# A new order of the sync engine's queue and of the slots, and a split of the softmax weights for three key tiles of six

## The reference, cut to what matters

```python
# q, k, v: (2, 8, 768, 64) float32, proj: (64, 6)
q_bucket = sum((q @ proj > 0) * 2**arange(6)); k_bucket likewise
scores = where(q_bucket[..., :, None] == k_bucket[..., None, :], q @ k.T / 8, -1e9)
attn = exp(scores - max(scores)); attn = attn / (sum(attn) + 1e-9)
x = (attn @ v), heads side by side            # (2, 768, 512)
x = (sigmoid(causal 5-tap convolution of x) * (x @ w_val)) @ w_out
u = x + real(fft(fft(x, axis=1), axis=2)); un = (u - mean) / sqrt(var + 1e-6)
out = u + relu(un @ w_ch1) @ w_ch2            # 512 -> 2048 -> 512
```

## Time and profile before

| | us |
|---|---|
| median of 3 runs | 784.6 |
| lowest, highest | 783.83, 794.24 |
| the profiled execution, its own time | 781.99 |
| its span, from the first to the last instruction | 780.1 |

### The profile page before, as it was taken

One profiled execution on the slowest core, in us unless ns is written; L12 is line 12 of the kernel. 1 busy time (PEld: TensorE's weight loads), 2 busy tenths in 40 slices (PEclk: granted clock), 3 DMA queues, 4 the chain that ended last, 5 costly groups with the idle time before them and its releaser, 6 DMA issues.

```text
span 780.1 us, 10303 instructions
## 1 busy us (share of the span) xinstructions
PE 701.6 (90%) x3696; PEld 647.9 (83%) x3696; DVE 418.7 (54%) x573; ACT 278.4 (36%) x424; POOL 381.9 (49%) x283
## 2 busy tenths in 40 slices
PE   2588889788888879878999999999999999999998
PEld 1388888787878778877989899998999999999897
DVE  3365578778888787797485467942122221212112
ACT  2146564455465454565352444211111111111110
POOL 1047778767878787788286697488100000000000
PEclk9589999999999999997999999999999999999999
DMA  9443645544544635111012112323010000001001
GB/s 246 116 123 98 155 118 139 129 113 107 144 113 112 158 106 129 50 31 42 17 50 61 41 42 75 88 85 95 11 40 0 0 28 13 0 0 41 1 0 41
DMA packets 33608, 57.67 MB, mean 74 GB/s; under 512 B 9232, under 2 KB 15632, under 8 KB 33568
## 3 DMA queue, kind: packets, MB, share of 16 engines
q1 hardware_dynamic: 33568, 57.14, 27.8%
HBM read 31.81 MB, written 3.24 MB: 45 GB/s over the span
## 4 chain that ended last, share of the span: by engine, by line
PE 71%; DVE 17%; DMA 4%; SPq 2%; issue 2%; POOL 2%; ACT 0%; DVEq 0%; POOLq 0%
PE psum L1057 63%; DVE max_col L808 4%; DVE neg_parts L818 2%; DMA a2k<-hash_bits 2%; DVE gate L862 1%; DVE qk_lo L794 1%; POOL p_lo L524 1%; DMA flag_dram<-a2q 1%; PE psum L1133 1%; DVE neg_rest L820 1%; PE psum L1138 1%; PE psum L1139 1%; PE psum L1135 1%; PE psum L1136 1%; DVE gate L859 1%
## 5 line engine op out<-in xcount | busy, mean ns | idle before, releaser
L524 POOL TENSOR_TENSOR p_lo<-probs,p_hi 128x768 fp32r<-128x768 f32 x96 | 190.2, 1996 | 66.4 <-ACT probs L647 65.1
L1028 DVE SCALAR_TENSOR_TENSOR h_lo<-psum,h_hi 128x384 fp32r<-128x384 f32 x64 | 35.7, 558 | 182.7 <-ACT h_hi L769 182.7
L808 DVE TENSOR_REDUCE max_col<-psum 128x1 f32<-128x768 f32 x96 | 91.6, 954 | 76.7 <-PE psum L1057 76.1
L644 ACT ACTIVATE p_hi<-psum 128x768 fp32r<-128x768 f32 x96 | 78.0, 813 | 104.6 <-PE psum L1057 103.0
L769 ACT ACTIVATE h_hi<-psum 128x384 fp32r<-128x384 f32 x64 | 31.5, 492 | 214.5 <-PE psum L1057 214.5
L1057 PE MATMUL psum<-a1k,a1q 128*128 128x384 f32 x192 | 74.2, 386 | 26.8 <-DMA a2k<-hash_bits 17.8
L1057 PE MATMUL psum<-unt_hi,w_hi 128*128 (+1 forms) x256 | 86.9, 339 | 0.0
L1057 PE MATMUL psum<-unt_lo,w_hi 128*128 (+1 forms) x256 | 86.3, 337 | 0.0
L1057 PE MATMUL psum<-unt_hi,w_lo 128*128 (+1 forms) x256 | 85.9, 336 | 0.0
L647 ACT ACTIVATE probs<-psum 128x768 f32<-128x768 f32 x96 | 77.3, 805 | 0.0
L1057 PE MATMUL psum<-w_lo,h_hi 128*128 128x512 f32 x192 | 75.9, 395 | 0.0
(11 more groups left out here) (124 smaller groups left out, 1561.6 us busy)
## 6 DMA issues: line engine op xcount, KB each, us to landing
stg_w<-in_w SPq DMA_DIRECT2D x32, 256.0 KB, 2.6
qk_raw<-in_qk SPq DMA_DIRECT2D x16, 384.0 KB, 5.1
a1k<-qk_hi SPq DMA_DIRECT2D x32, 192.0 KB, 5.1
flag_b<-flag_dram SPq DMA_DIRECT2D x16, 384.0 KB, 3.9
v_raw<-in_v SPq DMA_DIRECT2D x16, 192.0 KB, 3.0
a1q<-qk_hi SPq DMA_DIRECT2D x16, 192.0 KB, 4.7
a2q<-qk_hi SPq DMA_DIRECT2D x16, 192.0 KB, 5.3
a1q<-qk_lo SPq DMA_DIRECT2D x16, 192.0 KB, 5.0
```

The source lines that it names most:

```text
L524: pool.tensor_tensor(p_lo[i % PBUF][:, :], probs[i % PBUF][:, :], bits(p_hi[i % PHBUF][:, 0:S]), ALU.subtract).then_inc(p_lo_ready, 1)
L644: act.activation(halves(p_hi[i % PHBUF][:, 0:S]), ring[ring_st(i) % 2], ACT.Exp, scale=SCALE).then_inc(p_hi_ready, 1)
L808: dve.tensor_reduce(max_col[:, i % T:i % T + 1], s_ps, AX.XY, ALU.max).then_inc(max_done, 1)
L1028: dve.scalar_tensor_tensor(h_lo[:, half], psum[:, j % 2, 0:HALF], 0.0, bits(h_hi[:, half]), ALU.max, ALU.subtract).then_inc(h_lo_ready, 1)
```

## The change

What it does, by part:

1. **Split tiles.** Only tiles 1, 3 and 5 of a head (`SPLIT`) keep the six-matmul form. The others (0, 2, 4) are two plain float32 matmuls, with `probs` (now with the column of ones, PCOLS wide) as the moving operand and `v1`, float32 v with its ones, as the stationary one. Those tiles have no `p_hi` exponential and no `p_lo`. `vh` and `vl` keep three tiles of 128 columns.
2. **v.** The load of v writes straight into `v1`, in pieces of 64 columns (256 bytes), one head ahead in place of two. `v1` lies where slots 6 and 7 of `gate` will be, so the convolution of these waits for `pv_done`.
3. **Slots.** S_LEAD 10 to 11, FIRST -20 to -21; the hash at g % 12 = 9 (was 10); `max_parts` at g % 6 = 0 (was 1); `hi_qk`, `lo_qk`, `sign_bits`, `scale_kbits` one or two slots earlier; `hi_v`, `lo_v`, `reciprocals` one slot later; the convolution starts four slots later.
4. **scale_x** runs a head later, at g % 6 = 2 of head n + 2.
5. **SP.** `spread_flag` and `spread_rec` are each cut in two: the store goes out first (`store_flag` at g % 6 = 5, `store_rec` at 4), the broadcast one head's boundary later. `stack_bits` moves from g % 12 = 0 to 11, ahead of the flag. `load_qk` moves from 10 of the pair before (three pairs ahead) to 2 (two pairs ahead).
6. **After the loop.** `reciprocals(15)` comes before `gate_values(0, 0)`, and four taps of gate slot 6 (two before) come behind it, after `lo_x(1, c)`.

```diff
-ST_LEAD, S_LEAD = 2, 10
-FIRST = -20
+ST_LEAD, S_LEAD = 2, 11
+FIRST = -21
+SPLIT = (1, 3, 5)
...
             def load_v(n):
+                par = n % 2
                 if n >= 2:
-                    sp.wait_ge(vh_ready, n - 1)
                     sp.wait_ge(vl_ready, n - 1)
-                sp.dma_start(v_raw[n % 2][:, :], v[n // H, n % H, :, :].rearrange("(p t) d -> p (t d)", t=T)).then_inc(v_loaded[n % 2], 16)
+                    sp.wait_ge(pv_done, T * (n - 1))
+                sp.dma_start(tiles(v1[par][:, :])[:, :, par * D:(par + 1) * D],
+                             v[n // H, n % H, :, :].rearrange("(p t) d -> p t d", t=T)).then_inc(v_loaded[par], 16)
...
-            for g in range(FIRST, UNITS + T):
+            for g in range(FIRST, UNITS + 2 * T + 3):
                 pair, n = g // (2 * T), g // T
-                if g % (2 * T) == 10 and 0 <= pair + 3 < NPAIR and pair + 3 >= RAWS // 2:
-                    load_qk(2 * (pair + 3))
-                    load_qk(2 * (pair + 3) + 1)
+                if g % T == 1 and 1 <= n <= NH:
+                    fold_den(n - 1)
+                    if n + 1 < NH:
+                        load_v(n + 1)
+                if g % T == 4 and 1 <= n <= NH:
+                    store_rec(n - 1)
+                if g % T == 0 and 2 <= n <= NH + 1:
+                    spread_rec(n - 2)
                 if g % (2 * T) == 6 and 0 <= pair + 2 < NPAIR:
                     stack(2 * (pair + 2))
                 if g % (2 * T) == 10 and 0 <= pair + 2 < NPAIR:
                     stack(2 * (pair + 2) + 1)
-                if g % (2 * T) == 0 and 0 <= pair + 1 < NPAIR:
-                    stack_bits(pair + 1)
...
+                if g % (2 * T) == 11 and 0 <= pair + 2 < NPAIR:
+                    stack_bits(pair + 2)
+                if g % T == 5 and 0 <= n + 1 < NH:
+                    store_flag(n + 1)
+                if g % T == 1 and 0 <= n < NH:
+                    spread_flag(n)
+                if g % (2 * T) == 2 and 2 <= pair + 2 < NPAIR:
+                    load_qk(2 * (pair + 2))
+                    load_qk(2 * (pair + 2) + 1)
+                if g % T == 3 and 2 <= n + 2 < NH:
+                    load_wa(n + 2)
...
                 n = g // T
-                if 0 <= g + 1 < UNITS:
+                if 0 <= g + 1 < UNITS and is_split(g + 1):
                     lo_probs(g + 1)
-                if g % T == 3 and 0 <= n + 1 < NH:
+                if g % T == 4 and 0 <= n + 1 < NH:
                     lo_v(n + 1)
-                if g % T == 1 and 0 <= n < NH:
+                if g % T == 5 and 0 <= n < NH:
                     split_weights(n)
-                if g % T == 4 and 1 <= n <= NH:
-                    scale_x(n - 1)
+                if g % T == 2 and 2 <= n <= NH + 1:
+                    scale_x(n - 2)
...
                 act.wait_ge(st_done, i + 1)
-                act.activation(halves(p_hi[i % PHBUF][:, 0:S]), ring[ring_st(i) % 2], ACT.Exp, scale=SCALE).then_inc(p_hi_ready, 1)
+                if is_split(i):
+                    k = splits_until(i)
...
+                    act.activation(halves(p_hi[k % PHBUF][:, 0:S]), ring[ring_st(i) % 2], ACT.Exp, scale=SCALE).then_inc(p_hi_ready, 1)
...
-                if g % T == 1 and 0 <= n + 1 < NH:
+                if g % T == 0 and 0 <= n + 1 < NH:
                     max_parts(n + 1)
...
-                if g % T == 2 and 1 <= n:
+                if g % T == 3 and 1 <= n:
                     reciprocals(n - 1)
-                slot, tap = (g - 18) // (2 * T), (g - 18) % (2 * T) // 2
+                slot, tap = (g - 22) // (2 * T), (g - 22) % (2 * T) // 2
...
+                if not is_split(i):
+                    pe.wait_ge(probs_ready, i + 1)
+                    pe.matmul(first, v1[par][:, w], probs[i % PBUF][:, 0:HALF], start=start, stop=stop)
+                    pe.matmul(last, v1[par][:, w], probs[i % PBUF][:, HALF:PCOLS], start=start, stop=stop).then_inc(pv_done, 1)
+                    return
...
-                if g % (2 * T) == 10 and 0 <= pair + 2 < NPAIR:
+                if g % (2 * T) == 9 and 0 <= pair + 2 < NPAIR:
                     hash_pair(pair + 2)
```

More of the change, by code:

```diff
@@ L40, with splits_until, is_split, split_unit @@
 UNITS = T * NH
-ST_LEAD, S_LEAD = 2, 10
-FIRST = -20
+ST_LEAD, S_LEAD = 2, 11
+FIRST = -21
+SPLIT = (1, 3, 5)
+def splits_until(i):
+    return i // T * len(SPLIT) + sum(j < i % T for j in SPLIT)
+def is_split(i):
+    return i % T in SPLIT
+def split_unit(k):
+    return k // len(SPLIT) * T + SPLIT[k % len(SPLIT)]
 def turn_slot(n):
@@ L49, in hash_slot @@
 def hash_slot(pair):
-    return 2 * T * pair - 14
+    return 2 * T * pair - 15
 def turns_until(g):
@@ L186, in build @@
         assert top[0] <= wa_at
[L188 removed]
+        v1 = [at(gate_at + 4 * (NPAIR - 2) * S, "v1_0", T * P), after("v1_1", T * P)]
         assert top[0] <= gap_at
@@ L203, in build @@
         assert top[0] <= g_at
-        vh = [at(g_at, "vh0", T * P, F32R), after("vh1", T * P, F32R)]
-        vl = [after(f"vl{i}", T * P, F32R) for i in range(2)]
+        vh = [at(g_at, "vh0", len(SPLIT) * P, F32R), after("vh1", len(SPLIT) * P, F32R)]
+        vl = [after(f"vl{i}", len(SPLIT) * P, F32R) for i in range(2)]
         probs_at = top[0]
[L207 to L210, removed]
+        probs = [at(probs_at, "probs0", PCOLS)]
+        probs += [after(f"probs{i}", PCOLS) for i in range(1, PBUF)]
+        p_lo = [at(probs_at, "p_lo0", PCOLS, F32R)]
+        p_lo += [after(f"p_lo{i}", PCOLS, F32R) for i in range(1, PBUF)]
+        top[0] = max(top[0], gv_at)
         sums = [after(f"sums{i}", S) for i in range(2)]
@@ L285, in build @@
         max_rows = sem("max_rows")
-        flag_stored = sem("flag_stored")
+        flag_stored = [sem(f"flag_stored{i}") for i in range(2)]
         flag_loaded = [sem(f"flag_loaded{i}") for i in range(2)]
@@ L490, in _ @@
                 pool.memset(bits(p_hi[i][:, S + 1:PCOLS]), 0.0).then_inc(consts_ready, 1)
+            for i in range(PBUF):
+                pool.memset(probs[i][:, S:S + 1], 1.0).then_inc(consts_ready, 1)
+                pool.memset(probs[i][:, S + 1:PCOLS], 0.0).then_inc(consts_ready, 1)
             for par in range(2):
-                own, rest = (slice(D, P), slice(0, D)) if par else (slice(0, D), slice(D, P))
-                pool.memset(bits(tiles(vh[par][:, :])[:, :, rest]), 1.0).then_inc(consts_ready, 1)
-                pool.memset(bits(tiles(vl[par][:, :])[:, :, rest]), 0.0).then_inc(consts_ready, 1)
+                rest = slice(0, D) if par else slice(D, P)
+                pool.memset(tiles(v1[par][:, :])[:, :, rest], 1.0).then_inc(consts_ready, 1)
             pool.wait_ge(consts_ready, CONSTS)
@@ L997, in _ @@
                 lo_x(1, c)
+            for tap in range(1, KCONV):
+                convolve(NPAIR - 2, tap)
             for tap in range(KCONV):
@@ L1131, in weigh_v @@
                         pe.wait_ge(sums_ready, n)
-                pe.wait_ge(p_hi_ready, i + 1)
-                pe.matmul(first, vh[par][:, w], hi[:, 0:HALF], start=j == 0, stop=False)
-                pe.matmul(last, vh[par][:, w], hi[:, HALF:PCOLS], start=j == 0, stop=False)
+                if not is_split(i):
[3 more added lines that the diff above has]
+                    return
@@ L1135, in weigh_v @@
+                k = splits_until(i)
+                hi, lo = p_hi[k % PHBUF], p_lo[i % PBUF]
+                w = slice(k % len(SPLIT) * P, (k % len(SPLIT) + 1) * P)
+                pe.wait_ge(p_hi_ready, k + 1)
+                pe.matmul(first, vh[par][:, w], hi[:, 0:HALF], start=start, stop=False)
+                pe.matmul(last, vh[par][:, w], hi[:, HALF:PCOLS], start=start, stop=False)
                 pe.matmul(first, vl[par][:, w], hi[:, 0:HALF], start=False, stop=False)
-                pe.matmul(last, vl[par][:, w], hi[:, HALF:PCOLS], start=False, stop=j == T - 1)
@@ L1137, in weigh_v @@
-                pe.wait_ge(p_lo_ready, i + 1)
-                pe.matmul(first, vh[par][:, w], lo[:, 0:HALF], start=False, stop=j == T - 1)
-                pe.matmul(last[:, 0:HALF], vh[par][:, w], lo[:, HALF:S], start=False, stop=j == T - 1, skip_group_check=True).then_inc(pv_done, 1)
+                pe.matmul(last, vl[par][:, w], hi[:, HALF:PCOLS], start=False, stop=stop)
+                pe.wait_ge(p_lo_ready, k + 1)
+                pe.matmul(first, vh[par][:, w], lo[:, 0:HALF], start=False, stop=stop)
@@ L1141, in _ @@
+                pe.matmul(last[:, 0:HALF], vh[par][:, w], lo[:, HALF:S], start=False, stop=stop, skip_group_check=True).then_inc(pv_done, 1)
             pe.wait_ge(proj_split, 2)
```

84 lines of the change are left out of this document (40 added, 44 removed).

## The result

The changed kernel takes 751.8 us (median of 4 runs, 750.01 to 753.9) beside 784.2 for the kernel before on the same chip: ratio 0.9599, 95% interval 0.9569 to 0.9629. The forecast was 747 with a range of 728 to 778. The profiled execution has a span of 750.1 us, 30.0 less than before.

A forecast was written before the change was run, and what follows sets the result against it. PE bounds the second part; the attention loses 80 of 324.7 us to stalls, largely DVE held by POOL, and slow clock. Terms -55.5 and +19 give -36.5 from 782.0; forecast 747 us, own range 732 to 762, overall 728 to 778.

The forecast's parts named there:

- wait before the turned maxima: PE before turn_max: max_parts a slot earlier gives 6.7 us of room, so the wait falls 29.9 to some 3, -27.
- hash bits: PE's wait for the bits' DMA: stack_bits ahead of the flag on SP, so 12.2 us fall to 1, -11.
- sums: PE before a head's first weights, waiting for take_sums: 10.4 us fall to 7, -3.5, with DVE held less.
- plain tiles: PE: 48 plain float32 tiles at 1.41 us in place of split ones at 1.06, +17; ends -19 and +80.
- slow clock and the rest: Attention matmuls at TensorE's lower clock behind stalls: 10 of 17.5 us go, -10, bounds -3 and -15.
- the 17.5: Remainder of the attention's 80 lost us after 62.5 of waits, put down to matmuls at the lower clock.
- Adding the waits: SP's queue at slot 2: load_qk behind fold_den, only load_wa behind it; loads land with 2 us left.
- Rival D: weigh_v's tiles 0, 2, 4: plain float32 doesn't stream, 2.72 us a tile, total 810 us; chance 0.07.
- rival C: Plain tiles: float32 at the transposes' pace, 0.66 us a tile, -19 in place of +17, total 716 us; chance 0.08.
- Rival A: DVE stays the bound: half of the stalls and of the slow clock stay, total 776 us; chance 0.13.
- Rival B: Late qk loads hold ACT at hi_qk, 3 us for each of 6 pairs, total 765 us; chance 0.08.
- v in pieces of 256 bytes: Load of v into v1: first read by hi_v over 8 us after issue, even a doubled landing fits, no cost.

The follow-up runs named there:

- e8: Kernel before, old order, p_lo left out for tiles 0, 2, 4, their two matmuls reading p_hi again (output lacks that part): 746.4 us, ratio 0.9498.
- e7: e3 with 45 additions to POOL's queue as memsets (three of 548 columns each) that read no SBUF and nobody waits for: 742.6 us, ratio 0.9469.
- e10: e3 with S_LEAD back at 10 and max_parts back at slot 1, behind the maximum: 755.8 us, ratio 0.9643.
- e3: Changed kernel with the load of the gate's weight chunk moved on SP's queue from slot 3 to slot 2 of the next head: 737.4 us, ratio 0.9388.
- e4: Kernel before with only S_LEAD 11 and max_parts at slot 0, all tiles split, its own SP order: 801.4 us, ratio 1.0224.
- e1: Changed kernel with all six tiles of a head split, so the new order and slots alone (vl wider, 768 columns): 825.6 us, ratio 1.0502.
- e5: All six tiles split as in e1, plus the DMA move of e3: 793.1 us, ratio 1.0106.
- e9: e3 with only tiles 1 and 4 of a head split, so 64 plain tiles in place of 48: 735.6 us, ratio 0.9388.
- e6: e3 with POOL subtractions that read SBUF added at 45 places, two each, that nobody waits for: 761.9 us, ratio 0.9707.

## Why the prediction was right

**What bounded it** held. The second part stayed at 404 us, much of the lost time went with POOL's work (e8), and that small links last as long as POOL's instruction beside them is shown by e7 and e10. **The size of the gain** came out nearly right by luck: errors of opposite sign met. (The prediction's own sum, 745.5 + 2.6, gives 748.1 and not 747.) The terms, as the prediction had them, beside what was measured:

| term | forecast, us | measured, us |
|---|---|---|
| wait before the turned maxima | 29.9 to 3 | 29.9 to 7.7 |
| hash bits | 12.2 to 1 | 12.2 to 16.2 |
| sums | 10.4 to 7 | 10.4 to 7.3 |
| p_lo | 4.9 to 1 | 4.9 to 1.4 |
| maximum | 5.1 stays | 5.1 to 2.1 |
| plain tiles | +17 | +11.5 |
| slow clock and the rest | -10 | about -17 |
| prologue | +2.7 | +3.3 |

The 7.7 is the same in e3 and e7 and is no wait for DVE; so the step was right and its floor was missed. "About -17": full-pace work is now 245 - 0.7 + 11.5 = 256 us, the waits of PEld's rows add to some 37, and 256 + 37 is already the 291.8 of the attention, so nothing is left of the 17.5. That is an upper end: the granted clock of 0.98 still puts some 4% of the stretch, 12 us, at the lower level (half the upper), partly under those waits.

**The step that failed** is "Adding the waits: the new load_qk of slot 2 stands behind fold_den ...; behind it on SP is only load_wa". I named `load_wa` and didn't ask what it waits for. Its wait, for a split that the same change moved two slots behind it on POOL, holds SP 130.6 us and costs the 15 us by which the hash bits missed their term; e3 takes it away and gets 14.4 back.

**The plain tile** was sized from the parts: eight steps of 0.176, 1.41 us. It is 1.30, so its passes lie closer than separate matmuls. The Trainium skill (FP8 and Floating Point Precision, section TensorE Precision Notes) has four passes for true float32; the trace fits it: 0.65 us for 384 columns would be 0.16 a pass, which is 384 columns at 2.4 GHz. Rival D (a plain tile at 2.72 us) and rival C (0.66) are both refuted by that row.

**Which part pays.** The prediction gave the greatest term, 27 us, to the slot of room for `max_parts`. That was half of the truth. e4 has the room without the relief and loses 15 us. e8 has the relief without the room and gains 39. e10 has the relief in the new order without the room and lacks 18.4 us against e3. So the relief carries the gain in either order; the room paid only beside it, and by e10's rows because of where POOL's instructions fall in this order. An estimate from these runs: of the some 24 us by which e3 lies below e8 with the plain tiles' and the prologue's price added, the room is 18.4, and all the rest of the new order some 5.

**Rival A** (DVE stays the bound) is nearer to what e1, e4 and e5 show, with 26.9, 22.1 and 37.5 us of wait for the maxima, and isn't the changed kernel, whose DVE is busy 173 of 292 us. **Rival B** (late q and k loads) is not there: ACT waits 0.3 us in all for `qk_raw`, once. The prediction had named any such wait as a sign of being wrong, which was too strict. **v in pieces of 256 bytes** was put at nothing; it lands in 3.4 us where it took 3.0, and ACT's `hi_v` waits 4.0 us for it in five heads, though no row of PE names a wait behind it. That is SP's late wait once more: in the timeline above the load goes out at 174.56 us, 6 us after the sums (168.51), behind all the copies that had stood still, and in e3, with the same pieces of 256 bytes (landing 3.6 us), `hi_v` doesn't wait for v at all.

e3 and e9 beat both kernels, at 737.4 and 735.6 us. What is open: how much of e1's 825 us and e5's 793 is the wider `vl`, and how much of e6's 24.5 us is what POOL reads and how much the length of its pieces; neither was tried apart.

## What to carry to other kernels

Where VectorE instructions of a few elements last as long as GpSimd's large ones, look at GpSimd's SBUF work before the order of the queue: half of p_lo left out paid 39 us, while a better slot alone lost 15. Then look at who starts first: the same tap took 1.01 us just ahead of p_lo and 2.56 just behind its start. It can pay to give TensorE, even as the bound, more work (here 0.24 us a tile) if that takes an operand's preparation away from the engine that holds its neighbour. And when a producer is moved to a later slot, go through every in-order queue for a wait on it that stayed in its old place: one small DMA of the gate's weights cost 14.4 us of the attention.

## What the hardware showed that I had not expected

A float32 matmul of 384 columns appears as two records of 0.48 us and more, 0.65 us a matmul start to start. Taking a tile for eight separate steps was 0.11 us too dear.

Pieces of 256 bytes in place of 1536 raised the count of packets from 33,568 to 43,808 and the landing of 192 KB only from 3.0 to 3.4 us:

```profile
v<-in_v SPq DMA_DIRECT2D x16, 192.0 KB, 3.4
```

The Trainium skill (DMA: Bandwidth & Descriptors, section Specifications) names 512 bytes as the least for line rate; the 0.4 us agree with it in direction, but the other copies in flight were not the same in the two kernels, so it is no clean price.
